# Expert weights' low parts subtracted by DVE alone, later weight loads issued by GpSimd, tile bounds read one at a time

## What is computed

```python
do_compute = x @ w_skip > 0
xc = x[do_compute]
e_idx = np.argmax(xc @ w_gate, axis=1)      # one expert for each token
gate_w = softmax(xc @ w_gate)[e_idx]
for e in range(8):                          # w1: 8 x 384 x 1024, w2: 8 x 1024 x 384
    mask = e_idx == e
    y[mask] = gate_w[mask, None] * (np.maximum(xc[mask] @ w1[e], 0) @ w2[e])
out[do_compute] = xc + y                    # the other tokens keep x
```

## Time and profile before

| | |
|---|---|
| median of 3 runs | 813.08 us (812.76 to 816.14) |
| the profiled execution, its own time | 818.62 us |
| span of the profiled execution | 817.0 us |
| PE busy (share of the span) | 775.0 us (95%) |
| PE weight loads | 668.8 us (82%) |
| DVE busy | 455.4 us (56%) |
| ACT busy | 325.3 us (40%) |
| GpSimd (POOL) busy | 279.8 us (34%) |
| mean granted clock of PE | 0.978 of full speed |

### The profile page before, as it was taken

How to read it: one execution, slowest core, us unless ns; L and a number is a source line. 1 busy time by engine, 2 the same in 40 slices (tenths; PEclk the granted TensorE clock), 3 DMA queues, 4 the chain that set the end, 5 groups by cost and what they waited for, 6 DMA issues and landing times.

```text
span 817.0 us, 15673 instructions
## 1 busy us (share of the span) xinstructions
PE 775.0 (95%) x5539; PEld 668.8 (82%) x5539; DVE 455.4 (56%) x733; ACT 325.3 (40%) x629; POOL 279.8 (34%) x280
## 2 busy tenths in 40 slices
PE   7879999999999998999999999999899999999884
PEld 4357788888888887888888898998799999999774
DVE  7757876766676665766586635334422244244841
ACT  1444443433343333433343324343422255255621
POOL 6366662222224220522142310282420025241840
PEclk9889999999999999999999999999899999999988
DMA  8762522422233223322232005344432136445610
GB/s 260 221 185 60 151 63 59 128 59 59 60 97 89 60 59 102 89 59 59 82 105 52 16 25 193 134 148 166 156 126 68 58 126 204 149 136 175 244 36 7
DMA packets 52351, 88.31 MB, mean 108 GB/s; under 512 B 5948, under 2 KB 33832, under 8 KB 52272
## 3 DMA queue, kind: packets, MB, share of 16 engines
q1 hardware_dynamic: 42192, 62.19, 26.6%
q0 software_dynamic: 5504, 16.44, 5.6%
q10 hardware_dynamic: 4576, 8.65, 3.1%
HBM read 72.98 MB, written 16.75 MB: 110 GB/s over the span
## 4 chain that ended last, share of the span: by engine, by line
PE 90%; issue 4%; DVE 3%; ACT 3%; DVEq 0%; POOL 0%; POOLq 0%; ACTq 0%
PE bank L567 26%; PE bank L569 24%; PE bank L568 24%; PE bank L617 3%; PE bank L825 2%; PE bank L662 2%; PE bank L646 2%; PE bank L697 1%; ACT spare L928 1%; PE bank L686 1%; PE bank L626 1%; PE bank L773 1%; PE bank L764 1%; PE bank L651 1%; PE bank L656 1%
## 5 line engine op out<-in xcount | busy, mean ns | idle before, releaser
L567 PE MATMUL bank<-wo_hi,h_hi 128*128 128x394 f32 (+1 forms) x576 | 202.1, 351 | 1.6 <-DVE h_lo L1396 1.5
L569 PE MATMUL bank<-wo_hi,h_lo 128*128 128x394 f32 (+1 forms) x576 | 196.6, 341 | 0.0
L568 PE MATMUL bank<-wo_lo,h_hi 128*128 128x394 f32 (+1 forms) x576 | 196.4, 341 | 0.0
L1282 DVE SCALAR_TENSOR_TENSOR hid<-bank,hid 128x512 f32<-128x512 f32 x96 | 65.1, 678 | 152.0 <-ACT hid L958 152.0
L958 ACT ACTIVATE hid<-bank 128x512 f32<-128x512 f32 x96 | 57.0, 594 | 168.3 <-PE bank L569 161.3
L567 PE MATMUL bank<-xt_hi,wi_hi 128*128 128x512 f32 x288 | 118.7, 412 | 2.2 <-issue 2.2
L1472 POOL TENSOR_TENSOR work<-work 112x512 f32<-112x512 f32 x24 | 28.4, 1185 | 257.5 <-DVE work L1108 248.3
L567 PEld LDWEIGHTS bank<-wo_hi,h_hi 128*128 128x128 f32 x576 | 109.1, 189 | 7.6 <-DVE h_lo L1396 2.2
L569 PE MATMUL bank<-xt_hi,wi_lo 128*128 128x512 f32 x288 | 113.5, 394 | 0.0
L568 PE MATMUL bank<-xt_lo,wi_hi 128*128 128x512 f32 x288 | 113.4, 394 | 0.0
L568 PEld LDWEIGHTS bank<-wo_lo,h_hi 128*128 128x128 f32 x576 | 109.1, 189 | 3.0
(11 more groups left out here) (143 smaller groups left out, 1264.7 us busy)
## 6 DMA issues: line engine op xcount, KB each, us to landing
work<-rkw SPq DMA_DIRECT2D x48, 192.0 KB, 3.6
spare<-rk_rows SPq DMA_DIRECT2D x23, 384.0 KB, 4.3
work<-v_rows SPq DMA_DIRECT2D x25, 192.0 KB, 3.9
work<-sorted_rows SPq DMA_DIRECT2D x24, 193.0 KB
work<-rkw SPq DMA_DIRECT2D x48, 96.0 KB, 3.2
x_cur<-sorted_rows SPq DMA_DIRECT2D x24, 192.0 KB
x<-w POOLq DMA_DIRECT2D x6, 768.0 KB, 6.3
work<-w ACTq DMA_DIRECT2D x6, 768.0 KB, 7.4
```

The source lines that it names most:

```text
L567: pe.matmul(ps, a_hi, b_hi, start=start, stop=False, skip_group_check=True)
L568: pe.matmul(ps, a_hi, b_lo, start=False, stop=False, skip_group_check=True)
L569: return pe.matmul(ps, a_lo, b_hi, start=False, stop=stop, skip_group_check=True)
L1282: dve.scalar_tensor_tensor(hid[:, f % 2, :], HID[f % 2][:, :], 0.0, hid[:, f % 2, :], ALU.max, ALU.mult).then_inc(sb_sq, 1)
```

## The change

- DVE subtracts the low parts of all four pieces of experts 1 to 7. Pieces 2 and 3 of expert e+1 come behind the first tile's `hidden_lo` in expert e; expert 1's come behind tile 2. GpSimd keeps expert 0's pieces.
- GpSimd issues all four loads of experts 3 to 7 (`load_after`), each behind a wait for the low part of the piece that it overwrites; ACT issues none.
- PE, DVE, ACT and GpSimd read two, two, one and one bounds after tile 2, and one more at the start of each expert.
- PE's wait for x2_dve moves behind `hidden_transpose(0)`.

```diff
         def expert_loaded(k, e):
-            if k < 2 or e < 3:
+            if e < 3:
                 return e_loaded[e % 2][k], 16 * (e // 2) + 16
-            return e_sent[e % 2][k - 2], 16 * ((e - 3) // 2) + 16
+            return e_sent[e % 2][k], 16 * ((e - 3) // 2) + 16
...
             pe.wait_ge(x2_act, 2 * C)
+            hidden_transpose(0)
             pe.wait_ge(x2_dve, 2 * C)
-            hidden_transpose(0)
             for g in range(1, AHEAD):
                 next_tile(0, 0, g)
             pe.wait_ge(counted, 1)
-            starts = tile_starts(mybir.EngineType.PE, 1, NE + 2)
-            next_tiles(0, 0, AHEAD, starts[1])
-            last_contract(0, 0, starts[1], starts[2])
+            bound = [0, 0, *tile_starts(mybir.EngineType.PE, 2, 2)]
+            next_tiles(0, 0, AHEAD, bound[2])
+            last_contract(0, 0, bound[2], bound[3])
             for e in range(1, NE):
-                expert(e, e % 2, starts[e - 1:e + 3])
+                bound += tile_starts(mybir.EngineType.PE, e + 3, 1)
+                expert(e, e % 2, bound[e:e + 4])
...
                     rows_hi(lo + 1)
-                if e + 2 < NE:
-                    for k in range(2):
-                        act.wait_ge(e_lo1, 2 * e + k + 1)
-                        expert_load(act, k, e + 2)
                 if more:
...
             act.wait_ge(counted, 1)
-            starts = tile_starts(mybir.EngineType.Activation, 1, NE + 1)
-            next_tiles(AHEAD, starts[1])
+            hi = tile_starts(mybir.EngineType.Activation, 2, 1)[0]
+            next_tiles(AHEAD, hi)
             for e in range(1, NE):
-                expert(e, starts[e], starts[e + 1])
+                lo, hi = hi, tile_starts(mybir.EngineType.Activation, e + 2, 1)[0]
+                expert(e, lo, hi)
...
-                dve.tensor_tensor(lo_part, raw, hi_part.bitcast(F32), ALU.subtract).then_inc(e_lo1, 1)
+                dve.tensor_tensor(lo_part, raw, hi_part.bitcast(F32), ALU.subtract
+                                  ).then_inc((e_lo1, e_lo2)[k // 2], 1)
...
                     hidden_lo(lo)
+                if e + 1 < NE:
+                    for k in range(2, PIECES):
+                        split_expert_lo(k, e + 1)
                 next_tiles(lo + 1, hi)
...
             for g in range(1, AHEAD):
                 next_tile(g)
-                if g == 1:
-                    for k in range(2):
-                        split_expert_lo(k, 1)
+                for k in range(2 * g - 2, 2 * g):
+                    split_expert_lo(k, 1)
...
-            def split_second(e):
-
-                for k in (2, 3):
-                    split_expert_lo(k, e)
-                for k in (2, 3):
-                    if e + 2 < NE:
-                        pool.wait_ge(e_lo2, 2 * e + k - 1)
+            def load_after(e):
+
+                if e + 2 < NE:
+                    for k in range(PIECES):
+                        pool.wait_ge((e_lo1, e_lo2)[k // 2], 2 * e + k % 2 + 1)
                         expert_load(pool, k, e + 2)
...
-            split_second(1)
-            starts = tile_starts(mybir.EngineType.Pool, 1, NE + 1)
-            send_tiles(AHEAD - 1, starts[1])
+            load_after(1)
+            hi = tile_starts(mybir.EngineType.Pool, 2, 1)[0]
+            send_tiles(AHEAD - 1, hi)
             for e in range(1, NE):
-                if e + 1 < NE:
-                    split_second(e + 1)
-                send_tiles(starts[e], starts[e + 1])
+                load_after(e + 1)
+                lo, hi = hi, tile_starts(mybir.EngineType.Pool, e + 2, 1)[0]
+                send_tiles(lo, hi)
```

More of the change, by code:

```diff
@@ L177, in build @@
         e_loaded = [[sem(f"e_loaded{n}_{k}") for k in range(4)] for n in range(2)]
-        e_sent = [[sem(f"e_sent{n}_{k}") for k in range(2)] for n in range(2)]
+        e_sent = [[sem(f"e_sent{n}_{k}") for k in range(4)] for n in range(2)]
         w_hi = sem("w_hi")
@@ L1445, in _ @@
                 next_tile(g)
-                if g == 1:
-                    for k in range(2):
-                        split_expert_lo(k, 1)
+                for k in range(2 * g - 2, 2 * g):
+                    split_expert_lo(k, 1)
             dve.wait_ge(counted, 1)
[L1450 to L1453, removed]
+            bound = [0, 0, *tile_starts(mybir.EngineType.DVE, 2, 2)]
+            next_tiles(AHEAD, bound[2])
+            with dve.If(bound[2] >= bound[3]):
+                output_rows(bound[2])
             for e in range(1, NE):
-                expert(e, starts[e - 1:e + 3])
+                bound += tile_starts(mybir.EngineType.DVE, e + 3, 1)
+                expert(e, bound[e:e + 4])
         @block.gpsimd
```

## The result

| | before | after |
|---|---|---|
| median of 4 runs each | 814.54 us (812.76 to 816.14) | 803.80 us (800.32 to 804.82) |
| profiled execution, its span | 818.62, 817.0 us | 804.51, 802.9 us |
| mean granted clock | 0.978 | 0.989 |

The ratio of the times is 0.9861, with a 95% interval of 0.982 to 0.9902: faster by 1.4%. The forecast was 796.8, its range 795.3 to 803.0; the time lies 0.8 us above the range. The profiled execution was forecast at 802.3 and took 804.51.

The account below looks back on a forecast made before the run. PE was taken to bound the kernel, with a floor of 9.56 us a tile and stalls in tiles 3, 21 and 22. 6.84 + 9.49 = 16.3 us off the 813.08 median gave 796.8, range 795.3 to 803.0.

Parts of the forecast that it names:

- The bound reads: Tile 3: PE reads two bounds instead of ten, its 4.0 us wait goes, 16.40 falls to 9.56 us; gain 6.84 us.
- The single reads: Expert starts: seven added PE reads of one value, 0.6 us each, hidden because PE's sequencer is ahead; cost zero.
- rival 2: Expert boundaries: the reads show because PE's sequencer is less far ahead; up to 4.2 us, 801.0; chance 0.07.
- The subtractions: Tiles 21 and 22: GpSimd's SBUF reads no longer lock DVE out; wo piece 1.75 us on DVE; gain 9.49 us.
- rival 1: One-tile experts: DVE becomes the bound if a wo piece takes over 1.90 us; 799 to 803.6; chance 0.13.
- Rival 4: Tiles 21 and 22 stay as they are because the lock isn't what stretched DVE; 806.2; chance 0.04.
- The loads: Experts 3 to 7: GpSimd issues groups of four, 3.2 us a group; expert 7's the tightest; taken as zero.
- Rival 5: Per-tile row loads: groups of four fill the DMA engines and PE idles; 30.4 us slower, 827.2; chance 0.03.
- Rival 3: Expert 7's loads come late because GpSimd's issue waits for DVE; PE idles about 3 us; 802.9; chance 0.07.
- The opening wait: Tile 0: PE's x2_dve wait moves behind the transposes, which start about 1.1 us earlier; gain zero.
- The sum against the median: Whole kernel: the 16.3 us worked out on the 818.62 us profile was subtracted from the 813.08 us median, giving 796.8.

Follow-up runs that it names:

- e1_bounds: The kernel before with only the reading of the bounds changed, on all engines, to that of the changed kernel; median 807.69 us, ratio 0.9913 to before.
- g2_gpsimd_lo: Changed kernel with a separate semaphore for the ring's load, but GpSimd again subtracts pieces 2 and 3 for experts 1 to 7; median 806.39 us, ratio 0.9916 to before.

## Why the prediction was wrong in size and right in kind

**The bound reads**: right. I had 6.84 us of gain and tile 3 at 9.56; it is 9.56. Put back alone the ten reads cost 6.7 us in the profile and 6.2 to 6.3 group against group. The single reads cost nothing (0.31 us each, no boundary grew), as in the forecast and against rival 2. That PE reads two values in 0.72 us fits into the 2.7 us of cover; six at 2.09 don't.

**The subtractions**: right in mechanism and in DVE's price (1.72 us a wo piece, 1.75 forecast; rival 1 fell), wrong in size. "Gain 3.41 + 6.08 = 9.49 us" took two waits of one execution for the lock's price. Three profiles with these stalls and ACT's loads have 9.49, 8.4 and 6.26 us above the floor in tiles 21 and 22, by how the second meeting goes and by how far the clock falls behind it (0.78, 0.88, 1.00 in tile 22); with the loads on GpSimd the lock cost 4.85 in one profile and 7.0 between medians. What ordinary executions pay for lock and late load together can be estimated: without row waits the gain is 14.1 us (below); less 6.2 to 6.7 for the reads and 1.25 at the end, 6.1 to 6.7 are left, where I had 9.49; the intervals of the ratios leave 2 to 3 us of doubt in that. Rival 4, that the lock isn't the cause, fell with the memsets and with the lock put back alone.

**The loads**: "I take zero" was wrong twice, in opposite directions. Expert 7's pieces, issued by ACT, were too late once the lock was gone, so that 2.5 us of what I gave to the lock hang on the moved issue, and the groups of four cost 1.2 to 2.3 us by waits for rows. Only the second changes the sum, since the 2.5 us were in it already, under the wrong name. Rival 5 named this place and priced it at nothing below a landing of 8.6 us after the issue; the ring's load landed after 9.3, and cost 1.2 us in tile 4. I had read SP's wait of 6.6 us at four pieces in flight and not asked how near that is to 8.6. Rival 3 didn't come: GpSimd's issues take 0.77 to 0.80 us beside DVE's subtractions; its last one for expert 7 waits 1.18 us for the part that it replaces, and is in time.

**The opening wait**: zero, as forecast. From the ReLU at 530.09 us (531.21 after) to tile 1's transposes the two profiles have the same 43.6 us, though tile 0's transposes come 1.3 us earlier within it (1.1 forecast).

**The sum against the median**: the step that failed. "The floor and the waits are the kernel's own, so I take the same 16.3 off" put the stalls of one execution under a median of others. The term in it that was mis-sized is the 9.49 of the lock, 6.1 to 6.7 by the estimate above; the row waits, put at zero, took another 1.2 to 2.3. The miss of 7.0 us splits so: the profiled gain was 14.1 and not 16.3 (2.2: the row waits 2.3 and the early code 1.1, less the 1.25 at the end); the profiled execution of before stood 4.1 us above the median of its four runs, that of after 0.7 (3.4); and the median of before rose from 813.08 to 814.54 with the fourth run (1.5). That 4.1 had a sign in the numbers shown: 818.62 lay 2.5 us above the highest of the three runs, and I named the 5.5 and did nothing with it. The second profile of before names most of it: 3.2 us in tile 22, of which 2.4 are PE's work at the lower clock. (Both executions are of the later group in the early code, which lies above a median that falls between the groups.) With tile 22 at 12.4 the working would have been 13.1 us, and 800.0. That the gain is 1.25 us larger by the end of the span, which I had at nothing, is luck.

The larger counts agree with the smaller gain. The medians of before were 813.31, 815.12 and 814.62 us on three chips; the changed kernel's ratios were 0.9861 and 0.9858, so 11.5 us; with the row wait gone as well it is 0.9829 and 0.9824, so 14.1. The 95% intervals reach 2.0 to 3.4 us to either side, so the difference of 2.6 us is only in line with the row waits and doesn't prove them; the profiles do.

**Best version**: the changed kernel with a semaphore of its own for the ring's load. It is 1.7 to 1.8% faster than before. That it beats the changed kernel is shown by its profile, where the row waits are gone; the intervals of the two overlap.

What stays open: what makes the code before the experts take 3.4 us more in some executions, which of the two engines wins the lock, and why; what makes the end of the span 1.25 us shorter; and why the granted clock fell behind some waits of 2.4 us and not behind others.

## What to carry to other kernels

Before a stall's price goes into a sum, look how the profiled execution stands to the other runs: where it lies above all of them, its stalls are probably dearer than theirs, and a stall that hangs on two engines meeting is worth a range, not a number. Compare the mean granted clock too: here the profiled execution's was lower than in nearly all others. Where one cause of a wait is taken away, ask what it had hidden: here a late load stood behind the lock. And a wait that counts two transfers is as late as the one its engine doesn't need; give each its own semaphore before bursts of large loads are put in front of them.

## What the runs showed of the hardware that was not expected

- DVE and GpSimd, both with two inputs from SBUF, exclude each other, and either can be the one that waits: 8.80 beside 7.21 us in one execution, 6.29 and 2.92 beside 10.36 in another of the same kernel. A memset of GpSimd's doesn't take part (1.76 us).
- The same wait of PE has different prices, by the granted clock of its tile: waits of 2.33 to 2.40 us for xt_lo made a tile 3.4 us longer at 1.00 (both profiles of before, tile 21, with another 0.52 us of waiting for h_lo in it) and 4.2 to 4.3 longer at 0.88 (twice in e1_bounds, once in g2_gpsimd_lo). Behind waits of 3.95 to 4.14 us it was 0.79 in four profiles and 0.89 in one, behind 1.81 us 1.00.
- A row load of 192 KB lands in 2.3 to 2.6 us alone and in 6.3 to 9.3 behind four loads of 768 KB that run at 381 GB/s, with the second of two in a row the later one by 1 to 2 us.
- From tile 23's transposes to the end it is 16.7 to 16.8 us in the six executions in which ACT issues weight loads and 15.4 to 15.8 in the eight in which it doesn't. The last matmul ends 6.5 us behind those transposes in both, so the 1.25 us lie behind the last work that the profile shows. Why, no run asked.
- Runs of one kernel in which nothing stalls stand in two groups 3.4 us apart, and most of it arises in the first 60 us: the first ReLU begins at 56.2 us in two profiles and at 59.2 to 60.2 in the other twelve.
